# Attention's values products in one group, and the order of VectorE's and GpSimd's work beside them

## What is computed

```python
def _attn_ref(q, k, v, n_sink, window):          # q, k, v: (2, 8, 768, 64), n_sink 4, window 128
    scores = (1 / sqrt(D)) * q @ k.T
    keep = (pos_k < n_sink) | ((pos_q - pos_k >= 0) & (pos_q - pos_k < window))
    a = softmax(where(keep, scores, -1e9))
    return a @ v

def reference(...):
    x = attention, heads side by side             # 1536 tokens x 512
    x = moe(x)      # 8 experts of 192 tokens each, by greedy assignment of x @ w_gate;
                    # relu(x[mask] @ w1[e]) @ w2[e]
    h = x @ w_in;  return (max(h, 0) + alpha * min(h, 0)) @ w_out
```

## Time and profile before

| | |
|---|---|
| median of 3 runs | 635.93 us (635.57 to 637.14) |
| the profiled execution's own time | 635.48 us |
| its span, first to last instruction | 633.6 us |
| TensorE busy | 614.9 us, 97% |
| VectorE, ScalarE, GpSimd busy | 66%, 49%, 31% |
| TensorE's mean granted clock | 0.996 of 2.4 GHz |
| attention's last matmul (gate) | about 110 us after the start |

### The profile page before, as it was taken

How to read it: one execution, slowest core, us unless ns; L and a number is a source line. 1 busy time by engine, 2 the same in 40 slices (tenths; PEclk the granted TensorE clock), 3 DMA queues, 4 the chain that set the end, 5 groups by cost and what they waited for, 6 DMA issues and landing times.

```text
span 633.6 us, 12921 instructions
## 1 busy us (share of the span) xinstructions
PE 614.9 (97%) x4942; PEld 554.5 (88%) x4947; DVE 418.6 (66%) x1156; ACT 308.5 (49%) x716; POOL 196.5 (31%) x211
## 2 busy tenths in 40 slices
PE   8799999889999999999999999999999999999996
PEld 4689998759899888899999888999988989999995
DVE  7788887988576979844759797439687520035552
ACT  5888884512132655532236554322566542346663
POOL 5998881010121342111113421201233410113331
PEclk9999999899999999999999999999999999999999
DMA  7477754535450242037003510360017610000001
GB/s 261 152 260 273 276 192 161 190 96 198 140 204 1 68 171 104 2 114 264 14 2 103 204 37 2 137 254 1 2 67 246 243 64 13 1 1 1 1 1 50
DMA packets 31220, 72.36 MB, mean 114 GB/s; under 512 B 2876, under 2 KB 2936, under 8 KB 31160
## 3 DMA queue, kind: packets, MB, share of 16 engines
q1 hardware_dynamic: 27232, 60.69, 27.2%
q0 software_dynamic: 1984, 6.29, 3.0%
q10 hardware_dynamic: 1944, 4.56, 1.9%
HBM read 65.22 MB, written 6.32 MB: 113 GB/s over the span
## 4 chain that ended last, share of the span: by engine, by line
PE 78%; DVE 2%; issue 0%; ACT 0%; POOLq 0%; POOL 0%; DVEq 0%
PE bank L1602 22%; PE bank L1617 21%; PE bank L1514 14%; PE bank L1505 14%; PE bank L1392 3%; PE bank L1483 1%; PE bank L1461 1%; DVE beats L971 1%; DVE beats L942 0%; PE bank L1418 0%; PE bank L1445 0%; PE bank L1233 0%; PE bank L1438 0%; PE bank L1394 0%; DVE in_slot L1055 0%
## 5 line engine op out<-in xcount | busy, mean ns | idle before, releaser
L603 POOL TENSOR_TENSOR wi_lo<-w_in,wi_hi 128x512 fp32r<-128x512 f32 x64 | 89.0, 1392 | 272.5 <-ACT wi_hi L744 272.5
L942 DVE TENSOR_SCALAR beats<-rank_row,key 128x512 bf16<-128x512 f32 (+11 forms) x144 | 92.6, 664 | 11.5 <-PE bank L1394 11.5
L1617 PE MATMUL bank<-wo_lo,g_hi 128*128 128x512 f32 x192 | 76.0, 396 | 0.0
L1617 PE MATMUL bank<-wo_hi,g_lo 128*128 128x512 f32 x192 | 75.7, 394 | 0.0
L1617 PE MATMUL bank<-wo_hi,g_hi 128*128 128x512 f32 x192 | 75.5, 393 | 0.0
L1215 DVE SCALAR_TENSOR_TENSOR g<-bank,g_neg 128x384 f32<-128x384 f32 x64 | 35.5, 555 | 52.8 <-ACT g_neg L796 52.8
L794 ACT ACTIVATE g_neg<-bank 128x384 f32<-128x384 f32 x64 | 31.4, 491 | 78.1 <-PE bank L1602 77.7
L1602 PE MATMUL bank<-y_hi,wi_hi 128*128 128x384 f32 x256 | 57.9, 347 | 0.0
L770 ACT ACTIVATE h_t<-bank 128x192 f32<-128x192 f32 x64 | 21.2, 331 | 72.8 <-PE bank L1505 72.8
L670 ACT ACTIVATE prob<-neg_s,neg_max 128x260 f32<-128x260 f32 x96 | 48.8, 509 | 15.0 <-DVE neg_max L853 12.9
L1602 PE MATMUL bank<-y_lo,wi_hi 128*128 128x384 f32 x256 | 55.2, 336 | 0.0
(11 more groups left out here) (180 smaller groups left out, 1359.6 us busy)
## 6 DMA issues: line engine op xcount, KB each, us to landing
w_a<-moe_w SPq DMA_DIRECT2D x8, 1024.0 KB, 5.1
w_a<-moe_w SPq DMA_DIRECT2D x4, 2048.0 KB, 10.3
w_b<-moe_w SPq DMA_DIRECT2D x8, 1024.0 KB, 5.1
w_b<-moe_w SPq DMA_DIRECT2D x4, 2048.0 KB, 10.2
k_raw<-k_t SPq DMA_DIRECT2D x11, 512.0 KB, 5.3
q_raw<-q_t SPq DMA_DIRECT2D x11, 512.0 KB, 4.0
w_in<-moe_w_in SPq DMA_DIRECT2D x8, 512.0 KB, 5.0
w_out<-moe_w_out SPq DMA_DIRECT2D x8, 512.0 KB, 4.5
```

Of the source, the lines that this page charges most:

```text
L603: nc.gpsimd.tensor_tensor(out=wi_lo[:, f % 2, :, :], in0=w_in[:, :, f * P:(f + 1) * P], in1=wi_hi[:, f % 2, :, :].bitcast(F32), op=ALU.sub ...
L942: return nc.vector.tensor_scalar(out=beats[:, c % 3, lo:hi], in0=rank_row[:, lo:hi], scalar1=key[:, c:c + 1], scalar2=None, op0=op)
L1617: last = nc.tensor.matmul(DOWN_BANK[t][:, :], a[:, f % 3, t * P:(t + 1) * P], w[:, f % 2, :], start=(f == 0 and n == 0), stop=(f == FC - 1 ...
```

## The change

Three edits:

1. TensorE: all four pairs of values products of a step are issued together at head 1 of the slot in which it is `end`, instead of pairs 0 and 1 at head 7 of the slot before and pairs 2 and 3 at head 1.
2. VectorE: `normalise(late, 0)` with its reduction goes from head 0 to head 1, behind the second maximum; the sum of exponentials with its reciprocal goes from head 2 to head 1, ahead of the copy of pair 0.
3. GpSimd: the rounding of the next q goes ahead of packing the sinks, with one more wait, on its own earlier `qk_split`. ScalarE's order is unchanged: the rounding of k stood first in its slot before as well.

```diff
             def attention_slot(s):                      # GpSimd
                 mid, nxt = s - 1, s + 1
-                if 1 <= mid < STEPS:
-                    pack_sinks(mid)
                 if nxt < STEPS:
                     b, i = step(nxt)
                     pool.wait_ge(q_loaded[b], 16 * (i + b))
                     if nxt >= 2:
                         pool.wait_ge(scored, H * (nxt - 1))
+                    if nxt > 2:
+                        pool.wait_ge(qk_split, nxt - 1)
                     round_q(nc.gpsimd, nxt).then_inc(q_hi_done, 1)
+                if 1 <= mid < STEPS:
+                    pack_sinks(mid)
+                if nxt < STEPS:
                     pool.wait_ge(q_hi_done, nxt)
...
-                    if h == 0 and 0 <= late < STEPS:    # VectorE
+                    if h == 1 and 0 <= late < STEPS:
                         b, i = step(late)
                         dve.wait_ge(turned, 2 * late + 2)
                         chain.after(normalise(late, 0))
...
-                        if h == 2:
+                        if h == 1:
                             dve.wait_ge(exped, H * (mid + 1))
                             chain.after(nc.vector.tensor_reduce(out=p_add[:, :], in_=p_sum[b][:, :, :], axis=AX, op=ALU.add))
                             nc.vector.reciprocal(p_inv[b][:, :], p_add[:, :]).then_inc(sums_read, 1)
...
                     if h == 1 and 0 <= end < STEPS:     # TensorE
-                        values(end, 2)
-                        values(end, 3)
+                        for r in range(PAIRS):
+                            values(end, r)
...
-                    if h == 7 and 0 <= mid < STEPS:
-                        values(mid, 0)
-                        values(mid, 1)
```

## The result

The changed kernel takes 634.85 us (median of 20 runs, 633.63 to 637.08). The kernel before took 636.76 beside it (20 runs, 635.52 to 638.01). The ratio is 0.9977 with an interval of 0.9969 to 0.9985: 0.23% less, about 1.5 us, real but smaller than the 0.3% that counts as a change here. The medians themselves are 1.9 us apart; I go by the ratio. The prediction was 634.1, a gain of 1.8. The three runs that it started from had a median of 635.93, 0.83 lower than the 636.76 here, and the medians of before in the later comparisons are 636.24 to 636.51. So the 0.75 us between forecast and median come from the base.

The account below looks back on a forecast made before the run. TensorE, busy for 97% of the span, was taken as the bound. Slot 6's 0.62 plus 2.04 from slots 6 to 11 minus the tail's 0.88 gave 1.78 us gained: 634.1 us, range 633.0 to 636.1.

Parts of the forecast that it names:

- The gaps: TensorE, values products: two tile-shape gaps of 0.17 us fewer a slot, period 7.61 to 7.27; slots 6 to 11 gain 2.04.
- The tail: Slot 12 and behind: all four groups of step 10 now lie there, giving back 0.88 us (bounds 0 to 1.1).
- Rival 4: Tail's 0.88 is covered and GpSimd's idle time goes: 2.86 us gained, 633.1; chance 0.12 with other larger gains.
- Slot 6: Start of slot 6, set by GpSimd's rest of q: 55.27 instead of 55.89, 0.62 us gained.
- its order changes within a slot, not its sum: GpSimd, early slots: reordering costs nothing, so the starts of slots 3 and 4 stay.
- The open gain of 0.20: GpSimd's idle time before packing behind the first mask: if rounding q fills it, slots 4 to 12 start 0.20 us earlier.
- The first of these halves: Step 0's values half, moved out of slot 1, lay under GpSimd's time there and cost nothing.
- The feeders: VectorE, ScalarE and GpSimd keep up with the 7.27 us slot, with 0.05 to 0.2 us of room; costed at nothing.
- Rival 1: Feeders, not TensorE, set the period: at 7.40 us the gain is 1.0, time 634.9; chance 0.15.
- Rival 3: Gaps stay because each product's own wait makes them: period stays 7.61, only the tail is paid, 636.8; chance 0.04.
- Rival 2: VectorE's full queue delays a slot's last maximum: gain gone if 0.5 us late, 638.1 if 0.86 late; chance 0.07.
- q's rounding: GpSimd's moved cast: free in its new place; by slot 1's 1.39 us, slots 2 and 3 start 0.34 later each, gain 1.1.

Follow-up runs that it names:

- e5: Changed kernel with one full-width (128x128) product of zeros between pairs 1 and 2 of each values group: 637.62 us, ratio 1.0021.
- e6: Changed kernel with one 128x64 product of zeros, the values products' shape, between pairs 1 and 2 of each group: 635.53 us (one run).
- e4: Changed kernel with its group of four values pairs cut in two by the product that turns the sinks: 643.28 us, ratio 1.0114.
- e3: Changed kernel with step 0's values pairs 0 and 1 put back at head 7 of slot 1: 634.14 us, ratio 0.9973.
- the clean version: Changed kernel with step 0's values pairs 0 and 1 back in slot 1, timed twice: 634.14 us (0.9973) and 634.63 us (0.9972).
- e12: Changed kernel run again unedited, beside the version with step 0's first values group in slot 1: 635.37 us, ratio 0.9983.
- e1: Changed kernel run once more, unedited, for a second profile: 635.17 us, ratio 0.9976.
- e7: Changed kernel with GpSimd's old order, packing the sinks before rounding q: 636.1 us, ratio 1.0001.
- e9: Changed kernel with step 0's pairs 0 and 1 in slot 1 and GpSimd's two later masks built at program start: 633.8 us, ratio 0.996.

## Why the prediction came out right

**The gaps.** Right to the hundredth: period 7.26 to 7.27, 12 entries for 22, head 2 at T + 3.03. The Trainium skill, TensorEngine Tiling (Array Packing), Key Properties, says that changing the tiling mode drains TensorE. The traces agree that the gap goes with the change: e5 has one more, e6 with its narrow product none, 0.17 us at full clock, and 0.33 at the lower level in the changed kernel's first profile. The rule has a drain at each change; in e5 the change back in leaves 0.02. That fits a drain that is as short as the work in flight (16 columns there, 128 in e4 with 0.13), but no run varies the columns alone. Six periods in e3 save 45.66 - 43.60 = 2.06, predicted 2.04.

**The tail.** From slot 12's start to the end mark 7.28 before and 8.21 in e3 (slot 12 at 92.05 + 7.27 = 99.32): 0.93 paid, predicted 0.88. Rival 4 is out.

**Slot 6.** This is the mis-sized term: 55.27 predicted, 55.72 in e3, so 0.17 us gained and not 0.62. The step that failed is "its order changes within a slot, not its sum". Here is GpSimd in e3 from slot 3 to slot 5:

```profile
34.33 1.04 POOL L348 CAST q_hl<-q_raw 128x1024 fp32r<-128x1024 f32 x1 [0.21 <-issue]
35.31 0.51 POOL L531 COPY sink_p<-prob 128x32 f32<-128x32 f32 x3
36.00 2.39 POOL L366 TENSOR_TENSOR k_lo<-k_raw,k_hi 128x1024 fp32r<-128x1024 f32 x1 [0.18 <-POOL sink_p L531]
...
41.00 1.04 POOL L348 CAST q_hl<-q_raw 128x1024 fp32r<-128x1024 f32 x1 [0.16 <-POOL q_hl L359]
```

and the cast and both rests at the same place before, with the packing of slot 4 behind them:

```profile
34.66 1.04 POOL L348 CAST q_hl<-q_raw 128x1024 fp32r<-128x1024 f32 x1
35.78 2.39 POOL L366 TENSOR_TENSOR k_lo<-k_raw,k_hi 128x1024 fp32r<-128x1024 f32 x1
38.25 2.37 POOL L359 TENSOR_TENSOR q_hl<-q_raw,q_hl 64x1024 fp32r<-64x1024 f32 x1
40.74 0.51 POOL L531 COPY sink_p<-prob 128x32 f32<-128x32 f32 x3
```

From packing to the rest of k were 1.57 us (35.78 - 34.21); from the cast to it are now 1.67 (36.00 - 34.33). In both orders the rest of k waits by a semaphore for the instruction just in front of it. Behind the cast it started 0.08 us after its end (35.78 - 35.70), behind the packing it starts 0.18 after (36.00 - 35.82). That is 0.10 in each of slots 3, 4 and 5. The new wait on qk_split leaves 0.16 us in front of the cast where GpSimd comes to it without idle time, but the packing that stood there before waited for the same thing and had 0.12 (40.74 - 40.62), so it costs 0.04. I had counted both as nothing. Over slots 3 to 5 GpSimd needs 0.33 us more. The other 0.12 of the 0.45 is that slot 3 began later, at 32.48 and not 32.37; 0.09 of this is the same change in slot 2. The open gain of 0.20 did not come, since the idle time behind the mask stands there as before (0.21).

Together in e3: 0.17 + 2.06 - 0.93 = 1.30 us, the distance of the end marks. The timed ratios of the clean version are 0.9973 and 0.9972, about 1.7 us, and those of the changed kernel 0.9977, 0.9976 and 0.9983, 1.1 to 1.5 us. Marks and times are 0.4 us apart because the two profiled executions are only 1.38 apart (635.48 and 634.10): the one of before is one of its quickest.

**Luck.** The gaps and the tail were worked out and came. That the time came so near the forecast is in part luck: by the rows the clean version has 1.30 us of the 1.78, and in the changed kernel the fall of the clock comes on top, with end marks 0.92 ahead of before (e12), 0.52 ahead (e1) and 0.29 behind (the first profile). The range held because it was wide enough for other reasons.

**The clock.** No step of the prediction thought of it. "The first of these halves lay under GpSimd's time in slot 1, where it cost nothing" holds for the time of the products themselves (e3's slot 2 starts at 24.57, the changed kernel's at 24.64); whether taking them away lowers the clock behind them is likely, as said above, not shown.

**The feeders.** Rival 1 did not come: ScalarE, VectorE and GpSimd close where the rows put them, with 0.21 us left. Rival 3 fell with the first profile. Of Rival 2, no run made VectorE late. e7 makes the same loop late on GpSimd's side, and there the lateness is paid once in two slots. If that holds for VectorE's side too, Rival 2's price was doubled: 0.5 us late, less 0.2 of room, would cost 0.15 a slot and not 0.30.

**q's rounding.** It takes 1.04 us in its new place. The 1.39 of slot 1 is still there in the changed kernel, beside VectorE's subtraction of q, from 14.76 to 15.96. In e9 the cast comes later, at 15.61, when that subtraction is nearly over:

```profile
15.61 1.06 POOL L348 CAST q_hl<-q_raw 128x1024 fp32r<-128x1024 f32 x1 [0.39 <-POOL k_lo L366]
```

By the Trainium skill, GPSIMD Engine Reference, Specifications, GpSimd contends with VectorE instructions that have two SBUF inputs. The trace agrees where the cast starts within such an instruction: 1.39 us with 0.49 us of it left (15.47 to 15.96), 1.27 with 0.36 left in e12, 1.06 with 0.16 left in e9, 1.04 elsewhere. In e1 the subtraction began 0.50 us after the cast (15.15), beside its second half, and the cast took 1.04.

## What to carry to other kernels

Where gaps without a semaphore stand around one kind of matmul, count the changes of tile shape, and put all matmuls of that shape in one piece; where the matrix engine bounds the stage, the saving is the number of changes by the gap. When an engine's instructions change places and it bounds the stage, the short idle times between them change too, with what stands behind what, and tenths add up over the stage. Before moving work out of a stretch where the matrix engine mostly waits, look at its granted clock there in several executions: work that costs no time may still bear on what the engine is granted next (likely here, not shown).

## What the runs showed of the hardware

- TensorE's granted clock falls to half level once between 15 and 31 us in the ten profiles without the first values group, five times ahead of its place and five times behind it; the same kernel (after, e1, e12) shows both. By slot 6's start, against e3's, it costs between nothing (e6, 55.52) and 1.6 us (after, 57.31 against 55.72).
- A gap on leaving 128x64 tiles, 0.17 us (e5), and on going back 0.13 behind a product of 128 columns (e4) but 0.02 behind one of 16 (e5).
- Half the price for a late feeder whose loop spans two slots: 0.37 us late, 0.20 a slot (e7).
- The idle time of GpSimd in front of an instruction that waits for the one just before it differs with the pair: 0.08 us for the rest of k behind the cast, 0.18 behind the packing, 0.12 for the packing and 0.16 for the cast behind the rest of q (before, e3).
